# Routed expert stage: 31 tiles of 256 slots against 23 tiles of 256 and nine of 128, with a third weight buffer

## What is computed

```python
for t in range(S):                                   # attention, B=4 H=8 S=768 D=48
    state = alpha[:, :, t, :, None] * state + k_t v_t
    y[:, :, t] = einsum('bhd,bhde->bhe', q[:, :, t], state)
for e in range(8):                                   # dense experts, N=3072 D=384 F=1024
    out += P[:, e:e + 1] * (maximum(x @ w1[e], 0) @ w2[e])
noisy_logits = x @ w_gate + log1p(exp(x @ w_noise)) * noise
top2 = argpartition(-noisy_logits, 2, axis=1)[:, :2]     # weights: softmax over the two
for e in range(8):                                   # routed experts
    for k in range(2):
        mask = top2[:, k] == e
        out[mask] += top2_w[mask, k, None] * (maximum(x[mask] @ w1[e], 0) @ w2[e])
```

## Time and profile before

| | us |
|---|---|
| median of 3 runs | 2433.34 (2432.67 to 2436.16) |
| the profiled execution | 2441.35 |
| its span, first to last instruction | 2439.5 |

### The profile page before, as it was taken

One profiled execution on the slowest core, in us unless ns is written; L12 is line 12 of the kernel. 1 busy time (PEld: TensorE's weight loads), 2 busy tenths in 40 slices (PEclk: granted clock), 3 DMA queues, 4 the chain that ended last, 5 costly groups with the idle time before them and its releaser, 6 DMA issues.

```text
span 2439.5 us, 41923 instructions
## 1 busy us (share of the span) xinstructions
PE 2352.1 (96%) x14791; PEld 2343.3 (96%) x14791; DVE 1092.7 (45%) x1929; ACT 694.9 (28%) x1247; POOL 487.4 (20%) x307
## 2 busy tenths in 40 slices
PE   7999999999999999999999999999983999999998
PEld 7999999999999999999999999999982999999998
DVE  9972444333323333333233333333453666666664
ACT  3541111111111111111111111111441555555554
POOL 3332202022020220201202102022135232222222
PEclk9999999999999999999999999999995999999999
DMA  6561000000000000000000000000322577777775
GB/s 147 118 183 52 26 0 26 0 26 6 19 26 0 26 26 0 26 0 26 26 0 26 0 26 26 0 26 3 63 29 82 173 239 213 230 214 229 221 227 135
DMA packets 49056, 178.02 MB, mean 73 GB/s; under 512 B 15328, under 2 KB 33760, under 8 KB 39040
## 3 DMA queue, kind: packets, MB, share of 16 engines
q1 hardware_dynamic: 34592, 153.15, 20.5%
q0 software_dynamic: 14432, 24.44, 4.4%
HBM read 154.12 MB, written 23.45 MB: 73 GB/s over the span
## 4 chain that ended last, share of the span: by engine, by line
PE 91%; DVE 4%; issue 2%; DMA 1%; POOL 1%; ACT 1%; another core or an unknown queue 0%; DVEq 0%; ACTq 0%; SPq 0%; POOLq 0%
PE bank L1097 44%; PE bank L1088 43%; PE bank L1205 1%; DVE inv L681 1%; PE bank L1006 1%; DVE decay L675 1%; PE bank L1024 1%; DVE probs L688 1%; DMA slots<-record,places 1%; PE bank L1144 0%; POOL slots L435 0%; PE bank L1138 0%; PE bank L1021 0%; DMA qka_sb<-qka 0%
## 5 line engine op out<-in xcount | busy, mean ns | idle before, releaser
L1097 PE MATMUL bank<-w_hi,h_hi 128*128 128x384 f32 x2032 | 685.8, 338 | 4.2 <-DVE h_lo L761 4.2
L1097 PE MATMUL bank<-w_lo,h_hi 128*128 128x384 f32 x2032 | 680.7, 335 | 0.0
L1097 PE MATMUL bank<-w_hi,h_lo 128*128 128x384 f32 x2032 | 680.1, 335 | 0.0
L543 ACT ACTIVATE h_hi<-bank 128x384 fp32r<-128x384 f32 x512 | 251.5, 491 | 1325.3 <-PE bank L1088 1312.0
L1088 PE MATMUL bank<-x_hi,w_hi 128*128 (+1 forms) x1536 | 516.6, 336 | 0.0
L1088 PE MATMUL bank<-x_lo,w_hi 128*128 (+1 forms) x1536 | 515.6, 336 | 0.0
L1088 PE MATMUL bank<-x_hi,w_lo 128*128 (+1 forms) x1536 | 515.6, 336 | 0.0
L761 DVE SCALAR_TENSOR_TENSOR h_lo<-bank,h_hi 128x384 fp32r<-128x384 f32 x512 | 284.9, 558 | 381.5 <-ACT h_hi L543 365.6
L772 DVE SCALAR_TENSOR_TENSOR acc<-bank,route,acc 128x384 f32 (+1 forms) x336 | 186.8, 611 | 587.9 <-PE bank L1097 587.9
L1097 PEld LDWEIGHTS bank<-w_hi,h_hi 128*128 128x128 f32 x2032 | 382.3, 188 | 4.7 <-issue 4.7
L1097 PEld LDWEIGHTS bank<-w_lo,h_hi 128*128 128x128 f32 x2032 | 382.2, 188 | 0.0
(11 more groups left out here) (156 smaller groups left out, 1950.9 us busy)
## 6 DMA issues: line engine op xcount, KB each, us to landing
raw<-wts SPq DMA_DIRECT2D x78, 1536.0 KB, 6.6
qka_sb<-qka SPq DMA_DIRECT2D x48, 290.2 KB, 4.8
out_dram<-zrow SPq DMA_DIRECT2D x1, 5376.0 KB, 17.7
v_sb<-v SPq DMA_DIRECT2D x24, 192.0 KB, 2.5
x<-acc SPq DMA_DIRECT2D x8, 576.0 KB
xg<-x,slot_in POOLq DMA_INDIRECT x62, 6.0
out_dram<-ys,slot_out POOLq DMA_INDIRECT x62, 7.1
x<-zrow SPq DMA_DIRECT2D x1, 768.0 KB, 18.6
```

The lines of the kernel that those rows point to most:

```text
L543: act.activation(h_hi[:, f], ps_h[f][:, 0:TW], ACT.Relu).then_inc(s_hh, 1)
L1097: mm = pe.matmul(ps_o[s][:, 0:DM], hx, w, start=(first and n == 0), stop=(last and n == 2))
```

## The change

- `SUBS` lists the tiles: five of two blocks, then nine times (two, two, one). That is 32 tiles with 55 blocks in place of 31 with 62. `PAIRS` = 23 and `SINGLES` = 9. A tile of one block has up products with a moving operand of 128 tokens, half the down products, one gather and one scatter.
- The plan gives each expert its blocks as pairs first; what is left over after 23 pairs, and odd blocks, go to the singles. It has more and wider steps, and its index tables are made by more operations at the program's start (Pool `iota`, VectorE copies).
- Any expert may come first: tile 0 takes its expert and its slots from the plan, and its units take the common path. SP's loop for `raw` ends two units earlier, Pool's splits of those two units go, and ScalarE and VectorE split them.
- `raw2` has three buffers in turn; unit n uses buffer n mod 3, and its load waits for the split of unit n - 3.
- In front of the stage SP waits for the end of the dense products and the plan, loads unit 0, waits for the lists, and then issues both slot lists of the gathers, one of the outputs, and units 1 and 2.
- The turns of the next tile are in the first half of every tile, tile 0 too. The wait for the low turned rows before them is one wait.

The core of the diff:

```diff
-RW = 256
-RS = RW // P
+RS = 2
+RW = RS * P
-TILES = (2 * N - E) // RW + E
+HEAD, CYCLE = (2,) * 5, (2, 2, 1) * 2
+SUBS = HEAD + (2, 2, 1) * 9
+TILES = len(SUBS)
+PAIRS, SINGLES = SUBS.count(2), SUBS.count(1)
+RAWS = 3
-        raw2 = sb("raw2", [P, 2, W1C + W2C])
+        raw2 = sb("raw2", [P, RAWS, W1C + W2C])
@@ sync
-            with sp.Fori(1, E * 2 + 2) as u:
+            with sp.Fori(1, E * 2) as u:
+            def prefetch(tile, following, later):
+                expert, row = expert_of(following), first_slot(following)
+                if later is not None:
+                    later_expert, later_row = expert_of(later), first_slot(later)
+                sp.wait_ge(s_wl, 4 * tile.t + 2)
+                load_unit(following, expert, 1)
+                if later is not None:
+                    sp.wait_ge(s_gt, following.blocks + PRIMED)
+                    load_slots(later, later_row, slot_in, s_slot)
+                sp.wait_ge(s_free, tile.t + 2)
+                load_slots(following, row, slot_out, s_slo)
+                if later is not None:
+                    sp.wait_ge(s_wl, 4 * tile.t + 4)
+                    load_unit(later, later_expert, 0)
+
+            sp.wait_ge(s_od, 2 * E * TS * FC + PRIMED)
+            sp.wait_ge(s_plan, 1)
+            expert, row = expert_of(Tile(0)), first_slot(Tile(0))
+            next_expert, next_row = expert_of(Tile(1)), first_slot(Tile(1))
+            load_unit(Tile(0), expert, 0)
             sp.wait_ge(s_list, 32 * TT)
+            load_slots(Tile(0), row, slot_in, s_slot)
+            load_slots(Tile(1), next_row, slot_in, s_slot)
+            load_slots(Tile(0), row, slot_out, s_slo)
+            load_unit(Tile(0), expert, 1)
+            load_unit(Tile(1), next_expert, 0)
@@ gpsimd
-            split_unit(2 * E, 0)
-                    if t == TT - 2 * SUB:
-                        split_part(2 * E + 1, 1, 0)
+            def step(tile, following, later):
+                if later is not None:
+                    fetch(later, following.blocks)
+                scatter(tile)
-            split_part(2 * E + 1, 1, 1)
@@ scalar
+            def step(tile, following, later):
+                for half in range(2):
+                    n = 2 * tile.t + half
+                    for f in range(FC):
+                        act.wait_ge(s_ph, n * FC + f + 1)
+                        act.wait_ge(s_dn, n * FC + PRIMED)
+                        act.activation(h_hi[:, f, 0:tile.width], ps_h[f][:, 0:tile.width], ACT.Relu).then_inc(s_rh, 1)
+                    unit = (tile, following)[half]
+                    if unit is not None:
+                        high_weights(unit, 1 - half, 0)
+                    if half == 0 and following is not None:
+                        take_tokens(following)
+                    if unit is not None:
+                        high_weights(unit, 1 - half, 1)
@@ tensor
+            def step(tile, following, later):
+                for half in range(2):
+                    pe.wait_ge(s_wl, 2 * n + 1)
+                    pe.wait_ge(s_gl, tile.blocks + tile.subs + PRIMED)
+                    for f in range(FC):
+                        up(f, *w1, lambda k: xg_hi[:, tile.p, k, cols], lambda k: xg_lo[:, tile.p, k, cols],
+                           tile.width).then_inc(s_ph, 1)
+                    if half == 0 and following is not None:
+                        turn_gathered(following)
+                    pe.wait_ge(s_wl, 2 * n + 2)
```

More of the change, by code:

```diff
@@ L44, with __init__, follow @@
 PRIMED = 1
+RAWS = 3
+class Tile:
+    def __init__(self, o, turn=0):
+        past = SUBS[:o]
+        self.p, self.subs, self.width = o % 2, SUBS[o], SUBS[o] * P
+        self.t = o + len(CYCLE) * turn
+        self.blocks = sum(past) + sum(CYCLE) * turn
+        self.mine = sum(past[o % 2::2]) + sum(CYCLE) // 2 * turn
+        self.rank = o // 2 + len(CYCLE) // 2 * turn
+        self.raw = [(2 * o + half) % RAWS for half in range(2)]
+        self.load = [(2 * o + half) // RAWS + 2 * len(CYCLE) // RAWS * turn for half in range(2)]
+        self.pick = past.count(2) + CYCLE.count(2) * turn if self.subs == 2 else \
+            PAIRS + past.count(1) + CYCLE.count(1) * turn
+def follow(engine, step):
+    for o in range(len(HEAD)):
+        step(Tile(o), Tile(o + 1), Tile(o + 2))
+    with engine.Fori(0, TURNS) as turn:
+        for o in range(len(HEAD), len(HEAD) + len(CYCLE)):
+            step(Tile(o, turn), Tile(o + 1, turn), Tile(o + 2, turn))
+    for o in range(len(HEAD) + TURNS * len(CYCLE), TILES):
+        step(Tile(o), Tile(o + 1) if o + 1 < TILES else None, Tile(o + 2) if o + 2 < TILES else None)
 class Steps:
@@ L289, in first_slot @@
             def first_slot(tile):
[L290 to L297, removed]
@@ L324, in _, with load_slots @@
[L324 to L330, removed]
+                return sp.value_load(plan[0:1, 0, bass.ds(tile.pick, 1)], min_val=0, max_val=RI)
+            def load_slots(tile, row, buffer, loaded):
+                sp.dma_start(buffer[:, tile.p, 0:tile.subs].rearrange("p s w -> p (s w)"),
+                             slots[bass.ds(row, tile.width)].rearrange("(p s) w -> p (s w)", p=P))\
+                  .then_inc(loaded[tile.p], 16)
@@ L923, in _ @@
[L923 to L928 removed]
+            chosen_by, blocks, pairs, used, singles, first, ones_of = (count[:, n] for n in (0, 1, 2, 3, 4, 6, 7))
@@ L954, in run_step @@
-                    if half == turn_half(tile) and not last:
-                        low_tokens(tile + 1, 1 - p)
-            low_tokens(0, 0)
-            run_step(0, 0, False)
-            run_step(1, 1, False)
-            with dve.Fori(1, TILES // 2) as pair:
-                for p in range(2):
-                    run_step(2 * pair + p, p, False)
-            run_step(TILES - 1, 0, True)
+                    unit = (tile, following)[half]
+                    if unit is not None:
+                        low_weights(unit, 1 - half, 0)
@@ L1230, in _ @@
-            turn_gathered(0, 0, 0)
-            run_step(0, 0, False)
-            run_step(1, 1, False)
-            with pe.Fori(1, TILES // 2) as pair:
-                for p in range(2):
-                    run_step(2 * pair + p, p, False)
-            run_step(TILES - 1, 0, True)
+                        down(f, *w2, half == 0 and f == 0, half == 1 and f == FC - 1, tile.subs).then_inc(s_dn, 1)
+            pe.wait_ge(s_plan, 1)
+            turn_gathered(Tile(0))
+            follow(pe, step)
```

274 lines of the change are left out of this document (128 added, 146 removed).

## The result

| | before | after |
|---|---|---|
| median of 11 runs each, same chip | 2435.08 us (2430.57 to 2437.62) | 2438.58 us (2436.35 to 2448.03) |
| ratio after to before | | 1.0023, 95% interval 1.0015 to 1.0031 |
| profiled execution, its span | 2441.35, 2439.5 | 2436.75, 2435.0 |
| mean granted TensorE clock | 0.985 | 0.979 |

The change makes the kernel slower, by 0.23%; 2429.3 us and 4 us less were forecast.

The account below looks back on a forecast made before the run. TensorE was taken to bound the routed stage. Front +3.5, tiles -5.1 and end -2.4 us summed to -4.0, carried to the median of 2433.34: 2429.3 us, own range 2423 to 2439, over the cases 2420 to 2456.

Parts of the forecast that it names:

- The tiles: Routed stage: 23 two-block and nine single tiles, singles 15.54 us with waits for weights, 522.9 us instead of 527.9: -5.1 us.
- The rival of cheap products: Single tiles: 128-column products under 0.1 us, the gather then holds a single at 15.1 us; 2423.7 us in all, chance 0.10.
- plain f32: Rival in single tiles: narrow products run as plain f32 does, 0.224 us each; 2502 us in all, chance 0.14.
- 12.1 that TensorE's own work would make: Single tile: length in us from TensorE's work without waits, set against the 15.54 us forecast with waits for weights.
- The clock: Rival in single tiles: TensorE's clock falls after the new waits, 1.4 us lost per fall; 2442 or 2455 us, chance 0.18.
- dense down products between the waits: Single tiles: the argument given against the clock falling after the new waits; no size of its own.
- The front: Ahead of the routed stage: list timing zero, first gather beside weight loads +3 us, index tables +0.5 us; together +3.5 us.
- Lists earlier: Ahead of the routed stage: without Pool's weight split, places, plan and lists come up to 3.2 us earlier; net taken as zero.
- the nearest row is a gather: Ahead of the routed stage: first weight load beside landing lists, priced from a gather's 3.03 against 6.0 us; up to 3 later.
- Gather to turn: Ahead of the routed stage: first gather shares DMA engines with two weight loads, 6.0 instead of 3.03 us, +3 us.
- Index tables at the start: Program start: VectorE converts more index tables on the chain that ends last there, +0.5 us (0 to 1.5).
- The end: After the last tile: one scatter instead of two, 1.9 us, and one output operation about 0.5 us less; -2.4 us.

Follow-up runs that it names:

- after_again: The changed kernel, unchanged, run again on another chip for a second trace: 2436.49 us, ratio 1.0026 to before.
- gather_first: After, but Pool issues the gather three tiles ahead before waiting for the scatter's landing, its slot list loaded one tile earlier: 2436.57 us, ratio 1.0023 to before.
- front_behind: After, but SP loads unit 0 behind the slot lists and waits for the first gather before units 1 and 2: 2429.59 us, ratio 1.0003 to before.
- pairs_xg192: After with 31 two-block tiles, no singles, xg_hi 192 past a multiple of 256, x_hi placed as in after: 2420.78 us, ratio 0.9969 to before.
- before_xg192: The kernel before with 192 unused bytes ahead of xg, putting xg_hi 192 past a multiple of 256: 2416.64 us, ratio 0.9944 to before.
- before_again: The kernel before, unchanged, run again for a second trace: 2429.93 us, ratio 1.0002 to before.
- before_xg36: The kernel before with 160 unused bytes ahead of xg, putting xg_hi 160 past a multiple of 256: 2433.86 us, ratio 0.9991 to before.
- second group: Five runs: padding ahead of xg in before and after; after without singles, with later front loads, or with a two-block last tile: 2433.83 to 2448.44 us.
- fourth group: Three runs of after: earlier gather; that plus earlier w1 splits in singles; both plus moved xg and later unit 0 load: 2436.57, 2410.68, 2398.22 us.

## Why the prediction was wrong

The forecast was -4.0 us, the medians are +3.5 apart. The tiles' mechanism and price held. Two steps failed: at the end one scatter less was counted as -2.4 us and nothing else there as changed (measured +1.0), and in front the small slot list queued behind the weight load that the change puts ahead of it was not in the sum at all (+3 to +4 us, of which earlier lists take back 3). About half of the miss of 7.5 us is in neither. It is in no sum of the profiled executions, and its cause is open but for a part that goes with the clock.

**The tiles, -5.1 forecast, -4.4 measured: right in size, with two unseen terms that nearly cancel.** Single tile 15.52 for 15.54, products 0.110 and 0.113 us for 0.112, the wait 15 times and up to 1.5 us for 18 times and up to 1.7, no gather late but by 0.3 us. The rival of cheap products is out, and so is plain f32. ("12.1 that TensorE's own work would make" is too low: 72 x 0.112, 4.16 of down products and 0.66 of turns are 12.9, and 13.1 were measured once nothing waited.) The Trainium skill (TensorE: Matmul & The Clock Gate, Back-to-back issue gap) has about 81 ns for such a pair; the trace has 110 here, and the columns/1.2 ns of its section LDWEIGHTS (loading the stationary operand), 107 for 128 columns, come nearer. Unseen were 3.7 us of gain from the place of `xg` (23 x 0.16), and 3.0 us of loss from two clock falls (1.4 and 1.6). What is left for the tiling alone is 4.4 - 3.7 + 3.0 = 3.7 us of gain without falls. Of the 1.4 us missing to 5.1, 1.0 are in the eight tiles behind a single: about 17.6 us, where other two-block tiles of after take 17.46.

**The clock, a rival with chance 0.18: it happened, at its own price.** 1.4 us for a fall was forecast, 1.4 to 1.6 measured; the traces of after, after_again, gather_first and front_behind have 1 to 3 in the stage, not nine. The argument against it, dense down products between the waits, did not hold the clock; whether it makes falls rarer no run shows. By itself it doesn't reach the slower side, which needed seven.

**The front, +3.5 forecast, about +4 to +5 measured** (from the last dense product to the first up product 48.9 to 50.4 us in the later traces of before, 53.6 in its first, and 52.7 to 57.0 in the ten traces that have the front of after). One of its terms was missing and one taken as zero. Lists earlier by 3 us (30.2 to 27.2 in the later traces), inside the bounds of 3.2 and 3 but taken as zero. Slot list to gather +3 to +4, not in the sum at all: the step "the nearest row is a gather" looked at the list writes that the weight load could delay, and not at the slot list queued behind that load. Gather to turn +3 to +4.6, for +3. Index tables at the start: +0.5 forecast, the first dense product is at 182.0 and 182.3 for 182.7 and 181.4, nothing to be seen. pairs_xg192 against before_xg192 prices the whole at +4.1 us.

**The end, -2.4 forecast, +1.0 measured.** The largest single miss, 3.4 us. The scatter saved is real; the DRAIN behind it, that the views of the profile used for the forecast don't list, took 3.3 us more.

**The sum.** Against the typical trace of before (before_again: 547.9 us of stage, 9.6 us from slot list to up product): front +4.1, tiling, place and falls -5.3 (after) and -6.3 (after_again), end +1.0, which is -0.2 and -1.2, or about 1 more with the mean front of the traces. Measured are +3.5 us by the medians and +3.7 to +7.5 by the interval of the ratio. So some 3 to 5 us are not in the profiled executions: the untraced ones of after lie up to 11 us above its traced one, and the traced one of after_again (2429.05, where before_again's has 2428.93) is the fastest of nine, 7.4 below their median; those of before_again are 5 us apart in all. A part goes with the clock: its mean is 0.982 in that fastest one, 0.979 in the median one and 0.973 in the slowest. An estimate from this case's rows: one fall of 6.8 us takes 3.4/2430 = 0.0014 off the mean, so these are two and six falls more, and at 1.5 us each 3 of the 7.4 us and 9 to 10 of the 14. The last dense unit is one place: 126.8 us in before_again and before_xg192, 127.5 to 128.5 in six others on the same two chips, 131.2 for after, 131.9 for before_xg36 and 136.0 to 140.0 for three variants of after on the second group's chip, where the fourth group has 127.8 to 130.7. What makes it longer stays open, as does where the clock falls in executions without a trace.

The weak step was method. The term that the whole argument rested on, the price of a narrow product, was right to 0.002 us; the terms that decided the sign were small ones costed by "nothing" or from one row: what stands in a queue, what stands behind the last transfer, and what a larger table moves in memory.

## What to carry to other kernels

A tile with less work on the bounding engine is only as short as the work beside it, so halve a tile only after its weights, its gather and its lists are ahead; here either of two edits alone lost or did nothing, and both together gave 26 us. Ahead of a small transfer that everybody waits for, look for what was put into the same queue. Before comparing two tilings, put the operands at the same addresses.

## What the runs showed of the hardware

- The start address of the moving operand changed the pace of float32r products. For 256 columns `xg_hi` at 0, 64, 160 and 192 past a multiple of 256 bytes gave 0.1196, 0.1176, 0.1187 and 0.1133 us; for 384 columns 192 and 0 gave 0.1733, 128 gave 0.1760. The remainder by 256 fits all traces; that it is this remainder, and not a relation to the weights' addresses, is not shown, since the weights lay at 0 past a multiple of 256 in all of them. Products of 128 columns took 0.110 us at 64 and at 192. It was worth 13 us in the kernel before.
- A weight load of 1.5 MB among landing indirect writes moved at 29 to 88 GB/s for 10 us with the DMA engines 30 to over 90% busy, and took 15.1 us to land; once the lists had landed, it and the loads behind it moved at 320 to 420 GB/s.
- A 2 KB slot list sent into the queue behind that load landed 0.17 us after it, 4.4 us after its own issue; with no load ahead of it 1.6 us (front_behind).
- Pool's last DRAIN took 2.68 us in the six traces with 62 blocks and 5.99 in the eleven with 55.
- Half way through a single tile TensorE waited 0.74 to 0.77 us (1.40 in the last), at its end 1.4 to 1.5. Behind 2 of the 9 waits half way came 6.8 us at 1.2 GHz in after, behind 1 of 9 in after_again, and behind none of the waits at the end.
